# Layer 2 of the first MLP as pairs of 64-row matmuls into two PSUM banks, added by VectorE

## Time and profile before

| | us |
|---|---|
| median of 3 runs | 1469.6 |
| the profiled execution | 1469.29 |
| its span | 1467.5 |
| TensorE matmuls, busy | 1454.6 (99%) |
| TensorE weight loads, busy | 1204.1 (82%) |
| VectorE, busy | 906.8 (62%) |
| ScalarE, busy | 505.1 (34%) |
| layer 2 (L528), matmuls busy | 151.1, 648 matmuls |

### The profile page before, as it was taken

The page is one execution under the profiler, slowest core; times in us unless marked ns, Lnnn a source line. Parts: engine busy times, 40 slices in busy tenths (PEclk is TensorE's granted clock), DMA queues, the critical chain, the costliest instruction groups (busy, mean ns, idle before and its releaser), DMA issues.

```text
span 1467.5 us, 23064 instructions
## 1 busy us (share of the span) xinstructions
PE 1454.6 (99%) x9492; PEld 1204.1 (82%) x9492; DVE 906.8 (62%) x1464; ACT 505.1 (34%) x888; POOL 24.7 (2%) x25
## 2 busy tenths in 40 slices
PE   7999999999999999999999999999999999999999
PEld 7988888888888878788888888888888888888887
DVE  6865554545454626255776767767776676767666
ACT  2421212122121212244444444444444444444443
POOL 1500000000000000000000000000000000000000
PEclk8999999999999999999999999999999999999999
DMA  9222222221301000153000010100001010010000
GB/s 343 84 84 85 77 67 73 64 84 34 105 30 60 30 29 2 52 178 115 1 29 29 1 58 1 58 0 29 29 0 58 0 43 15 8 50 1 29 1 29
DMA packets 34477, 75.74 MB, mean 52 GB/s; under 512 B 3152, under 2 KB 3152, under 8 KB 34384
## 3 DMA queue, kind: packets, MB, share of 16 engines
q1 hardware_dynamic: 34384, 74.46, 15.0%
HBM read 55.57 MB, written 18.87 MB: 51 GB/s over the span
## 4 chain that ended last, share of the span: by engine, by line
PE 94%; DVE 4%; issue 1%; DMA 1%; ACT 1%; SPq 0%; DVEq 0%; ACTq 0%
PE psum L514 28%; PE psum L578 26%; PE psum L561 26%; PE psum L528 10%; PE psum L497 2%; PE psum L473 2%; DVE probs L781 0%; DMA v_first<-in_v 0%; DVE probs L766 0%; DVE row_max L762 0%; DVE row_sum L773 0%; DVE h L813 0%; DVE g L850 0%; DVE best L807 0%; ACT h L643 0%
## 5 line engine op out<-in xcount | busy, mean ns | idle before, releaser
L514 PE MATMUL psum<-x,w 128*128 128x512 f32 (+1 forms) x2160 | 453.0, 370 | 1.3 <-DVE x L792 1.0
L514 PEld LDWEIGHTS psum<-x,w 128*128 128x128 f32 x2160 | 377.1, 190 | 72.0 <-issue 2.4
L578 PE MATMUL psum<-w_out_s,g 128*128 128x512 f32 x1728 | 415.0, 389 | 0.9 <-DVE g L850 0.9
L578 PEld LDWEIGHTS psum<-w_out_s,g 128*128 128x128 f32 x1728 | 324.1, 188 | 69.0 <-DVE g L850 1.7
L861 DVE SCALAR_TENSOR_TENSOR poly<-poly,u_sq 128x512 f32<-128x512 f32 x144 | 99.7, 692 | 235.8 <-ACT poly L695 235.8
L687 ACT ACTIVATE u_sq<-psum 128x512 f32<-128x512 f32 x144 | 86.1, 598 | 425.9 <-PE psum L561 425.9
L561 PE MATMUL psum<-x_odd,w_in_s 128*128 128x512 f32 x960 | 229.9, 389 | 0.0
L561 PEld LDWEIGHTS psum<-x_odd,w_in_s 128*128 128x128 f32 x960 | 180.2, 188 | 37.4
L561 PE MATMUL psum<-x_even,w_in_s 128*128 128x512 f32 x768 | 184.5, 389 | 0.0
L561 PEld LDWEIGHTS psum<-x_even,w_in_s 128*128 128x128 f32 x768 | 144.2, 188 | 30.0
L528 PE MATMUL psum<-h,w_mid_s 128*128 128x512 f32 x648 | 151.1, 391 | 0.9 <-DVE h L813 0.9
(11 more groups left out here) (48 smaller groups left out, 708.1 us busy)
## 6 DMA issues: line engine op xcount, KB each, us to landing
v_raw<-in_v SPq DMA_DIRECT2D x21, 512.0 KB, 4.5
q_t<-in_q SPq DMA_DIRECT2D x36, 256.0 KB, 3.6
x_scratch<-x_stage SPq DMA_DIRECT2D x36, 256.0 KB, 2.8
out<-out_stage SPq DMA_DIRECT2D x36, 256.0 KB, 2.1
k_raw<-in_k SPq DMA_DIRECT2D x28, 288.0 KB, 2.8
x_raw_odd<-x_scratch SPq DMA_DIRECT2D x5, 1024.0 KB, 5.2
w_raw<-in_w SPq DMA_DIRECT2D x6, 768.0 KB, 12.4
x_raw_even<-x_scratch SPq DMA_DIRECT2D x4, 1024.0 KB, 5.2
```

The lines of the kernel that those rows point to most:

```text
L514: mm = pe.matmul(psum[:, bank, 0:hi - lo], w123[:, m, ws, n, c, :], x[:, xs, c, lo:hi], start=(c == 0 and ws + xs == 0), stop=(c == KC1 - ...
L578: mm = pe.matmul(psum[:, j, :], g[:, m % 4, gs, j * P:(j + 1) * P], w_out_s[:, m, ws, :], start=(m == 0 and gs + ws == 0), stop=(m == MC2 ...
```

## The change

Each layer-2 matmul, which contracts over 128 rows, becomes two that contract over 64 rows each (partitions 0 to 63 and 64 to 127), issued one behind the other. They write to two banks of the ring. ScalarE copies the first bank to the staging buffer as before. VectorE then waits for that copy and for the second bank, adds that bank to the staging buffer in place, and only then may SP store it. Instructions on TensorE for layer 2: 1296 matmuls and as many weight loads instead of 648.

```diff
@@ USES
-        for _i in range(NW if _e[0] == "l1" else 1):
+        for _i in range(NW if _e[0] == "l1" else 2):
@@ SP
                 if entry[0] == "l2":
-                    bank, before = USES[entry][0]
+                    bank, before = USES[entry][1]
                     sp.wait_ge(drained[bank], before + 1)
@@
-            wait_filled(sp, ("l2", NT - 1, KC1 - 1))
+            for n in range(2):
+                wait_filled(sp, ("l2", NT - 1, KC1 - 1), n)
@@ TensorE, layer2
-                bank = open_bank(entry)
+                banks = [open_bank(entry, n) for n in range(2)]
                 for m in range(MC1):
...
                     for ws, xs in split_passes():
-                        mm = pe.matmul(psum[:, bank, :], w_mid_s[:, ws, m, c * P:(c + 1) * P], h1[:, xs, m, :],
-                                       start=(m == 0 and ws + xs == 0), stop=(m == MC1 - 1 and ws == 1))
-                mm.then_inc(filled[bank], 1)
+                        for n, bank in enumerate(banks):
+                            rows = slice(n * P // 2, (n + 1) * P // 2)
+                            mm = pe.matmul(psum[:, bank, :], w_mid_s[rows, ws, m, c * P:(c + 1) * P], h1[rows, xs, m, :],
+                                           start=(m == 0 and ws + xs == 0), stop=(m == MC1 - 1 and ws == 1))
+                            if m == MC1 - 1 and ws == 1:
+                                mm.then_inc(filled[bank], 1)
@@ VectorE
+            def add_x2(entry):
+                _, t, c = entry
+                e = t * KC1 + c
+                first, before = USES[entry][0]
+                dve.wait_ge(drained[first], before + 1)
+                bank = wait_filled(dve, entry, 1)
+                nc.vector.tensor_tensor(x2_stage[:, e % 2], psum[:, bank, :], x2_stage[:, e % 2], ALU.add)\
+                    .then_inc(drained[bank], 1)
@@ VectorE, walk of ORDER
+                if entry[0] == "l2":
+                    add_x2(entry)
```

## The result

The changed kernel takes 1473.01 us, the median of 9 runs (1472.29 to 1474.44), against 1469.2 for the kernel before (9 runs): a ratio of 1.0027, 95% interval [1.0017, 1.0038]. It is slower by about 3.8 us. The forecast was 1473.1.

What follows compares the result with a forecast made beforehand. The prediction took TensorE's matmul stream to bound the kernel. To the profiled 1469.29 us it added 0 for pairs, 3.4 for switches and 0.1 for late halves, giving 1472.8, or 1473.1 as a median; range 1465.6 to 1482.5.

Steps and rivals of the forecast that it cites:

- Part 1: Layer 2 on TensorE: a pair of 64-row matmuls takes 226.6 ns, as the full matmul does; change 0.
- the attention rounds: Attention product of tile 8: eight narrow float32 matmuls at once, 430 ns a round, 2 to 3 ns beyond streaming.
- the 13.3 ns: Time each full-array fp32r matmul takes beyond streaming its columns; 8.6 us in layer 2, forecast to stay once per pair.
- Rival A: Layer-2 pairs lose the overhead: 216 ns instead of 226.6, -7.0 us, 1466.1 us with the switches; chance 0.29.
- Part 2: Switches of the array's shape around layer 2: 18 new ones at 0.20 us, 3.4 us after tile 0's wait.
- my upper bound of 0.24: Most that one switch at a border of layer 2 costs: the dearer switch and a few slow matmuls behind it.
- 3.4 + 0.1: Layer-2 borders: 3.4 us for switches, 0.1 for second halves starting some 7 ns late at 18 ends of a stretch.
- Parts 3 and 4: VectorE's 36 additions (25 us) hide in idle time: 0. SP's store waits 0.7 us longer: 0, at most 6.
- C: Layer-2 pairs: two overheads add, or loads run in turn; 240 ns a pair, +8.6 us, 1481.7 us; chance 0.15.
- D: Layer-2 pairs do not overlap in fp32r: +147 us, 1620 us; chance 0.04.
- B: Switches around layer 2 cost nothing and the overhead stays: 1469.7 us, no change; chance 0.12.
- The 4 ns per further tile: Skill's rule for each further tile of a pack; by it layer-2 pairs would cost 2.6 us more.

Runs made afterwards that it cites:

- the quads: Layer 2 in four 32-row matmuls into four banks with three additions by VectorE, where the kernel before has full 128-row matmuls: 1579.72 us.

## Why the prediction was right

- **Part 1, the period of a pair.** The forecast of 226.6 ns came true (226.5), with the two halves 3 ns apart instead of the 7 I had taken from the attention rounds. But the reason I gave for it was half wrong. I said that the 13.3 ns go with fp32r; what the runs show is that bf16 pays nearly as much when the moving operand is read at full rate over 4-byte places (225 ns), and not when it lies densely (216). Nothing else differs between these two kernels' matmuls. That the same reading costs fp32r its 13.3 ns is the likely conclusion and not shown by itself, since an fp32r number always fills 4 bytes. The overhead hides at half rate (429) and at the half clock (427). What carried the forecast was the sentence behind it: per partition the halves read the same columns as before. Rival A read its 2 to 3 ns from float32 rounds, and these hid the overhead in their half rate, not in their narrowness. The one quantity that decides between A and the forecast had no row in the trace of before. (Rival A's -7.0 us is 648 x 10.8; by its own 216 and 226.6 it is 648 x 10.6 = 6.9.)
- **Part 2, the switches.** 0.20 us each was right for the gap itself and for both of its terms: 0.09 before the first pair and 0.11 by the second load. The slow matmuls behind, which stood only in my upper bound of 0.24, come every time, so a switch is 0.25 (0.49 us a tile with two). The sum would have been 17 x 0.25 = 4.2 instead of 3.4 + 0.1.
- **Why the total still fits.** The spans differ by 3.7. Nine tiles account for some 4.2, and the profiled execution happened to be some 0.5 us earlier at the first layer-2 entry (88.21 against 88.76 for the last layer-1 matmul before it). The forecast also started from a median of 1469.6 that 9 runs put at 1469.2. That the forecast of 1473.1 lies within 0.1 of the median of 1473.01 is therefore luck: two small errors cancel, and the same kernel gave +4.4 in its second comparison. In the runs above, the last matmul before the first layer-2 entry starts anywhere from 87.7 to 89.5 us, so half a microsecond there says nothing of the change. The medians' 3.8 against the predicted 3.5 is well within the interval of 2.5 to 5.6.
- **Parts 3 and 4, VectorE and SP.** 36 x 0.69 = 24.8 us, all hidden, as said; no wait of TensorE is put down to it. Tile 1's fourth addition starts at 182.46 and ends at 183.15, where 183.1 was forecast. The kernel with banks and additions alone shows it by itself (1.0003).
- **Rivals.** A pair at 226.5 ns rules out A (216), C (240) and D (no overlap), and the 0.20 us at each border rules out B (a switch costs nothing). The Trainium skill says that a change of the tiling mode drains TensorE (TensorEngine Tiling, Key Properties). The 0.09 us before the first pair would fit that; the other 0.11 follow the second load. The same page lists 64 columns at 128 rows as a configuration of its own (Available Configurations), and between it and 128 columns the trace shows no gap (0.226 us).
- **The 4 ns per further tile** that the skill's TensorE: Matmul & The Clock Gate (Part 3) has for a pack is there as 3 ns between the starts of the halves, but the period doesn't grow by it (226.5 ns against 226.6).

## What to carry to other kernels

Splitting a contraction that already fills the rows bought nothing: the halves stream side by side in the time of the whole, and each change of row shape cost TensorE 0.25 us with fp32r weights, so if narrow tiles are needed at all, count the borders and not the tiles. An overhead read from one kind of matmul (float32 at half rate) must not be carried to another (full rate) before one short run has shown it. Where split precision allows it, dense 2-byte moving operands give back 10.7 ns of every 512-column matmul, which with the shorter loads gave 8 us for a tenth of this kernel's matmul time.

## What the runs showed of the hardware

- A full-rate matmul of 512 columns comes each 226.7 ns with fp32r operands, 225 with a bf16 moving operand at a stride of two, and 216 with a dense one.
- After a switch of shape the second matmul comes 0.335 us behind the first with fp32r weights, whose second load starts 0.11 us behind the first, and 0.23 to 0.24 with bf16 weights, where it starts 0.015 behind.
- 32-row tiles of one round keep separate times: their starts lay up to 0.05 us apart at the full clock, and 0.11 in the round in which the clock fell.
- After TensorE was idle for 2.9 us at a time (the quads), the granted clock fell to 0.50 within 1.3 us of its next matmul.
